# Linear attention and two MLP layers in one kernel: the first layer's groups of three chunks become groups of 2, 4, 4, 4, 4, 4, 2

## What is computed

```python
for t in range(S):
    cur = np.einsum('bhd,bhe->bhde', u[None] * kt, vt)
    y[:, :, t] = np.einsum('bhd,bhde->bhe', rt, state + cur)
    state = w[None, :, :, None] * state + np.einsum('bhd,bhe->bhde', kt, vt)
```

```python
h = np.maximum(np.maximum(x @ w1, x @ w2), x @ w3); x = h @ w_out          # d_ff 768
xn = x / rms * rms_g; out = (silu(xn @ w_gate) * (xn @ w_val)) @ w_out     # d_ff 1536
```

## Time and profile before

| what | us |
|---|---|
| median of three runs | 871.98 (867.09 to 873.14) |
| the profiled execution, its own time | 867.5 |
| its span, first to last instruction | 865.8 |
| granted TensorE clock, mean over the span | 0.996 of 2.4 GHz |

### The profile page before, as it was taken

One profiled execution on the slowest core, in us unless ns is written; L12 is line 12 of the kernel. 1 busy time (PEld: TensorE's weight loads), 2 busy tenths in 40 slices (PEclk: granted clock), 3 DMA queues, 4 the chain that ended last, 5 costly groups with the idle time before them and its releaser, 6 DMA issues.

```text
span 865.8 us, 14428 instructions
## 1 busy us (share of the span) xinstructions
PE 838.9 (97%) x5480; PEld 734.3 (85%) x5480; DVE 361.6 (42%) x665; ACT 314.1 (36%) x684; POOL 148.7 (17%) x148
## 2 busy tenths in 40 slices
PE   3799999999999999999999999999999999999998
PEld 2599999999999999999788888888888888888886
DVE  7675445445535545335333423522433252343221
ACT  3743434243434334343545232332332323233212
POOL 6652321322312321003324000000000000000000
PEclk9899999999999999999999999999999999999999
DMA  6643123113213121032221000000000000000000
GB/s 236 200 162 111 54 68 92 57 59 104 59 53 111 53 79 33 4 96 73 57 71 37 1 37 1 0 37 1 1 22 14 0 0 36 0 0 37 0 1 37
DMA packets 45157, 45.40 MB, mean 52 GB/s; under 512 B 3504, under 2 KB 39728, under 8 KB 45104
## 3 DMA queue, kind: packets, MB, share of 16 engines
q1 hardware_dynamic: 45104, 44.65, 16.4%
HBM read 38.74 MB, written 4.72 MB: 50 GB/s over the span
## 4 chain that ended last, share of the span: by engine, by line
PE 93%; DVE 3%; ACT 1%; issue 1%; DMA 1%; SPq 1%; DVEq 0%; ACTq 0%
PE h_b L442 12%; PE h_b L444 11%; PE h_b L443 11%; PE h2y_b L442 8%; PE h2y_b L444 8%; PE h2y_b L443 8%; PE y_b L444 6%; PE y_b L442 6%; PE y_b L443 6%; PE at_b L403 3%; PE at_b L429 3%; PE at_b L444 3%; PE at_b L442 3%; PE at_b L443 3%; PE at_b L424 1%
## 5 line engine op out<-in xcount | busy, mean ns | idle before, releaser
L442 PE MATMUL h_b<-xh,Wh 128*128 128x384 f32 (+1 forms) x396 | 144.4, 365 | 1.3 <-DVE hB L857 1.3
L444 PE MATMUL h_b<-xh,Wl 128*128 128x384 f32 (+1 forms) x396 | 139.2, 352 | 0.0
L443 PE MATMUL h_b<-xl,Wh 128*128 128x384 f32 (+1 forms) x396 | 139.0, 351 | 0.0
L753 ACT CAST hh<-hB 128x512 fp32r<-128x512 f32 x72 | 44.7, 621 | 163.0 <-DVE hB L1019 160.9
L748 ACT ACTIVATE hA<-h_b 128x512 f32<-128x512 f32 x72 | 43.1, 598 | 125.6 <-PE h_b L444 125.6
L444 PE MATMUL y_b<-hh,Wl 128*128 128x512 f32 (+1 forms) x240 | 88.2, 367 | 0.0
L442 PE MATMUL y_b<-hh,Wh 128*128 128x512 f32 (+1 forms) x240 | 88.1, 367 | 0.0
L443 PE MATMUL y_b<-hl,Wh 128*128 128x512 f32 (+1 forms) x240 | 88.1, 367 | 0.0
L442 PEld LDWEIGHTS h_b<-xh,Wh 128*128 128x128 f32 x396 | 74.7, 189 | 10.4 <-issue 2.8
L1019 DVE TENSOR_TENSOR hB<-h2y_b,hA 128x512 f32<-128x512 f32 x36 | 24.9, 691 | 137.5 <-PE h2y_b L444 137.5
L605 ACT ACTIVATE A<-hA,cur 128x128 f32<-128x128 f32 x192 | 60.6, 390 | 53.5 <-DVE cur L808 36.8
(11 more groups left out here) (151 smaller groups left out, 1553.3 us busy)
## 6 DMA issues: line engine op xcount, KB each, us to landing
kbuf<-in_kT SPq DMA_DIRECT2D x24, 256.0 KB, 3.5
rbuf<-in_rT SPq DMA_DIRECT2D x24, 256.0 KB, 3.5
rnbuf<-in_r SPq DMA_DIRECT2D x24, 192.0 KB, 2.5
knbuf<-in_k SPq DMA_DIRECT2D x24, 192.0 KB, 3.1
vbuf<-in_v SPq DMA_DIRECT2D x24, 192.0 KB, 3.6
x<-in_wA SPq DMA_DIRECT2D x6, 768.0 KB, 6.7
out_t<-xraw SPq DMA_DIRECT2D x5, 768.0 KB, 3.7
wst<-in_gv SPq DMA_DIRECT2D x6, 384.0 KB, 3.2
```

Of the source, the lines that this page charges most:

```text
L442: nc.tensor.matmul(bank[:, 0:n], hi, xhi, start=first, stop=False)
L443: nc.tensor.matmul(bank[:, 0:n], hi, xlo, start=False, stop=False)
L444: return nc.tensor.matmul(bank[:, 0:n], lo, xhi, start=False, stop=last)
L753: nc.scalar.copy(hh[:, f % 2, :], hB[:, f % 2, :]).then_inc(g_hi, 1)
```

## The change

Chunks c and slots q are now counted through the whole run (q = 2c and 2c + 1). Loops of layer 1 are written out.

```diff
-GC = 3
+SIZES = (2, 4, 4, 4, 4, 4, 2)
+NG = len(SIZES)
+STARTS = [sum(SIZES[:g]) for g in range(NG)]
+RING = 3
-SLOTS = (("w1",), ("w1",), ("w1",), ("w1",), ("w1", "out"), ())
+PLACES = {0: (),
+          4: ((0, "w1"), (1, "w1"), (2, "w1"), (3, "w1")),
+          8: ((0, "w1"), (1, "w1"), (1, "w3"), (2, "w3"), (3, "w1"), (3, "w3"), (4, "w1"), (4, "out"))}
+PLACES_0 = ((0, "out"), (1, "w1"), (1, "out"), (2, "w3"), (3, "w1"), (3, "w3"), (4, "w1"), (4, "out"))
+        ident = sb(att, "ident", [P, P])
+        mask = sb(att, "mask", [P, C])
+        p3 = sb(att, "p3", [P, max(SIZES), C])
```

```diff
 SyncE: loads and moves
-            for j in range(GC):
-                load_chunk(0, 0, j)
+            load_chunk(0)
+            load_chunk(1)
             load_wA(0)
             load_wA(1)
-            load_chunk(0, 1, 0)
+            load_chunk(2)
             load_wA(2)
-            move_p3(0, 0)
+            move_p3(sp, 0, HOLES[:3])
+            load_chunk(3)
             load_wA(3)
-            load_chunk(0, 1, 1)
+            load_chunk(4)
             load_wA(4)
             load_wA(5)
 GpSimd: prologue; the low parts of weights go
-            pool.wait_ge(u_loaded, 16)
-            for k in range(Q):
-                prep_r(0, 0, k, first=k < DUOS, following=(0, 1))
-                if k == 0:
-                    wA_low(1)
-                if k == 1:
-                    wA_low(2)
+            prep_r(0)
+            prep_r(1)
+            scale_k(0)
+            prep_r(2)
+            scale_k(1)
+            prep_r(3)
+            pool.wait_ge(u_loaded, 16)
+            current(SIZES[0])
 ScalarE: prologue
+            for q in range(Q0):
+                if q + 2 < Q0:
+                    diagonal(q + 2)
+                take_y(q, FIRST[q % 3])
+                if q == 1:
+                    wA_high(0)
+                if q == Q0 - 2:
+                    move_p3(act, 0, HOLES[3:])
             for c in range(KC):
-                x_high(0, 0, c)
+                x_high(0, c)
+            wA_high(1)
 ScalarE: group and tail
-                    if first and f + 3 < F1:
-                        for third in range(3):
-                            wA_high(f + 3, third)
                     copy_w1(g, f)
+                    if g == 0 and f == 0:
+                        diagonal(Q0)
+                        diagonal(Q0 + 1)
                     slot_work(f, "w1")
                     slot_work(f, "w2")
                     hidden_hi(g, f)
+                    slot_work(f, "w3")
                     slot_work(f, "out")
+                    if g == 0 and f + 2 < F1:
+                        wA_high(f + 2)
+                if f == 4:
+                    normed_high(0, PAR2)
                 for piece in EARLY_SPLITS[f]:
                     split_high(*piece)
-                if f == 4:
-                    normed_high(0, 0)
 VectorE: slot_work and group
+                if q + 1 < NQ:
+                    place_scores(q + 1, at_b)
+                sum_state(q, at_b)
+                if q % 2 == 0 and q // 2 + 1 < NCH:
+                    sum_current(q // 2 + 1)
+                if q + 2 < NQ:
+                    prep(q + 2)
                         if part == "w2":
+                            if g == 0 and f + 1 < F1:
+                                wA_low(f + 1)
                             maximum(g, f, 1)
 VectorE: prologue
             nc.vector.tensor_tensor(pw[:, 7, :], pw[:, 6, :], pw[:, 6, :], ALU.mult)
+            first_current(0)
             then(nc.vector.reciprocal(ipw[:], pw[:, 0:6, :]))
...
+            prep(0)
+            sum_current(0)
             nc.vector.tensor_tensor(PKw, PK[:, :, :].rearrange("p (h m) c -> p h m c", h=2),
...
             dve.wait_ge(consts_ready, 2)
-            prep(0, 0, 0)
-            sum_current(0, 0, 0)
-            prep(0, 0, 1)
-            place_scores(0, 0, 0, FIRST[0], 3)
+            prep(1)
+            first_current(1)
+            place_scores(0, FIRST[0], 3)
+            sum_current(1)
 VectorE: tail, layer 2's first norm
-                if f == 3:
+                if (f, part) == (3, "out"):
                     reciprocal_rms(0)
-                    normalise(0)
-                if f == 4:
-                    normed_low(0, 0)
+                if (f, part) == (4, "out"):
+                    normalise(0)
+                    normed_low(0, PAR2, (0,))
+                if (f, part) == (5, "w2"):
+                    normed_low(0, PAR2, (1, 2))
```

More of the change, by code:

```diff
@@ L652, in group @@
+            def group(g, tail=None):
+                work = slots(g)
+                def slot_work(f, part):
+                    if (f, part) in work:
+                        q = work[f, part]
+                        if q + 2 < NQ:
+                            diagonal(q + 2)
+                        take_y(q, at_b)
                 for f in range(F1):
-                    if f == F1 - 1 and ai is not None:
+                    if f == F1 - 1 and g + 1 < NG:
                         for c in range(KC):
-                            x_high(ai, apar, c)
@@ L886, in wA_low, with group @@
+            def wA_low(f, thirds=(0, 3)):
+                dve.wait_ge(wA_hi, 3 * f + thirds[1])
+                n = W1F // 3
+                cut = slice(f * W1F + n * thirds[0], f * W1F + n * thirds[1])
                 last = nc.vector.tensor_tensor(Wl[:, cut], wraw[:, cut], Wh[:, cut].bitcast(F32), ALU.subtract)
[L887 removed]
+                if thirds[1] == 3:
                     last.then_inc(wA_lo, 1)
[L890 to L893 removed]
+            def group(g, tail=None):
+                work = slots(g)
```

544 lines of the change are left out of this document (244 added, 300 removed).

## The result

In 16 executions of each, on the same chip, the kernel before took 869.91 us (867.09 to 873.14) and the changed one 876.56 us (873.36 to 878.15): a ratio of 1.0078, with a 95% interval from 1.0061 to 1.0094. It is slower by 0.8%, 6.7 us; the forecast was 2.0 above the 871.98 known then. The profiled execution has a span of 875.4 us (before 865.8, forecast 867.8), and a mean granted clock of 0.986. The two profiled executions are not the median ones: the one of before (867.5 us) lies 2.4 us under its median, that of the change (877.18) 0.6 over. So the spans are 9.6 us apart where the medians are 6.7 apart, and what follows accounts for the 9.6.

The account below looks back on a forecast made before the run. TensorE's stream was taken as the bound, busy for 97% of the span. 28.1 + 48.5 + 4 x 63.3 - 1.0 + 56.1 + 35.0 = 419.9 us, layer 2 -0.5, span 867.8, median about 874.0; range 859 to 886.

Parts of the forecast that it names:

- Group sizes: Layer-1 matmuls: 256 columns take 0.120 us each, so all layer-1 products cost 296.7 us, a gain of 2.7 us.
- Rival (b): Layer 1: weight loads set the pace of 256-column matmuls, at 0.173 us each the time is 887 us; chance 0.07.
- Slots and middle groups: Layer 1: two more slots in the groups +3.6 us, joined slots -1.2; a four-chunk group takes 63.3 us without stall.
- rival (e): Middle groups: eight slots don't fit, a miss of 1 us in each of five groups, 879 us; chance 0.10 with (d).
- Prologue: Start of the first group: two chunks instead of three bring the first product to 28.1 us, 9.1 us earlier.
- Rival (d): Start of the first group: the prologue gains nothing beyond 33 us, 879 us; chance 0.10 together with (e).
- First group: First 256-column group: 39.9 us of work plus 8.6 of TensorE waits, 48.5 us in all.
- rival (c): First group: the clock falls in its waits, 19 us more, half absorbed, 884 us; chance 0.05.
- Last group: Last 256-column group: 27.3 us of work plus waits of 1.9, 1.7 and 4.1, sum 35.0 us.
- Layer 2: After layer 1: layer 2 changes by one project, -0.5 us.
- The sum: Whole kernel: layer 1 ends at 419.9 us, where 417.42 was; span 867.8 us, median about 874.0.
- (a): First and last groups: waits stay at lower bounds, -6.2 and -4.4 us, 863.4 us; chance 0.28.

Follow-up runs that it names:

- all3: Changed kernel with eight groups of three chunks, its other edits kept and loads and slot places fitted: 872.74 us, ratio 1.0047.
- cur_pool: Changed kernel with first_current undone, GpSimd again making the products of chunks 0 and 1 in the prologue: 877.67 us, ratio 1.0111, four executions.
- fill_first: Changed kernel with idle 256-column matmuls in three TensorE waits: behind the prologue and ahead of two first-group slots: 872.91 us, ratio 1.0038.
- norm_early: Changed kernel with layer 2's first norm begun one group earlier: 865.71 us, ratio 0.9973.
- fill_end: Changed kernel with 20 idle 512-column matmuls ahead of TensorE's wait for the last maximum before layer 2: 873.57 us, ratio 1.0035.
- last3: Changed kernel with group sizes (2, 4, 4, 4, 4, 3, 3), so three chunks in the last group: 867.78 us, ratio 0.9993.
- gate_split: Changed kernel with TensorE's wait ahead of layer 2 divided, only the value products waiting for the last maximum: 873.7 us, ratio 1.0033.
- y_first: Changed kernel with ScalarE's take_y put ahead of the diagonals in the groups' slot work: 872.17 us, ratio 1.0044.
- first6: Changed kernel with sizes (2, 3, 4, 4, 4, 4, 3), so six slots in the first group: 867.63 us, ratio 0.9983.
- early_y_first6: Changed kernel with the edits of norm_early and y_first and the sizes of first6: 860.26 us, ratio 0.9905.

## Why the prediction was right, and where it wasn't

The time fell into the forecast's case (874.0 forecast, 876.56 measured, own range 866 to 880), within 1% of before and on its slow side. That closeness is partly luck. The 874.0 stood on a median of three, 871.98, which is 869.91 in 16 executions; the change itself was forecast at +2.0 us and measured at +6.7, and the span's sum missed 7.6 us. The range was wide enough for that. What failed is one mechanism, the clock behind TensorE's waits, which the sum put at nothing. By the steps of the prediction:

- **Group sizes: held.** 256 columns take 0.120 us, as assumed. Rival (b), loads that set the pace, is out. The five middle groups take 308.2 us, forecast 308.3.
- **Slots and middle groups: held.** There is no wait in 308 us, so rival (e), slots that don't fit, is out. Joining the rows of slots seems worth 0.4 us per group in all3, which has the other edits too, against the 0.2 assumed.
- **Prologue: held.** First product at 27.76, forecast 28.1. The copies were issued until 25.8 on ScalarE and 26.1 on SP, and the casts follow:

```profile
23.95 1.88 ACTq L241 DMA_DIRECT2D xraw<-p  x3
23.95 2.15 SPq L241 DMA_DIRECT2D xraw<-p  x3
...
27.44 0.71 ACT L621 CAST xh<-xraw 128x256 fp32r<-128x256 f32 x2 [0.29 <-DMA xraw<-p]
```

  What cur_pool adds: without first_current it would be 30.2. Rival (d) is out.
- **First group: two errors that half cancel.** The forecast was 39.9 of work and 8.6 of waits, 48.5; it was 51.0, inside the 45 to 52 that the prediction allowed. The waits are 4.7. At full clock they would be more, up to 6.6 by fill_first (its fillers and idle time together): the low clock stretches the parts between slots, and the chain behind a slot gains time by that. The step that failed is in rival (c), "against: the longest wait I find there is 3 us". A wait of 2.15 us was followed by 6.3 us at the lower level, and the prologue's pause, which I knew to end in a slow product, by 3.5 us of it, which the sum did not hold at all. 46.15 us busy at 0.87 are 40.1 at full clock, the forecast's 39.9: the work was sized right, and 6.0 us of clock were left out. fill_first shows the cause: with the clock kept up the group takes 3.6 us less. Rival (c) thus happened in part; its price of 19 us, half absorbed, was for a clock that stays down, and it came back each time. The rows of before held the term already: the 2.4 us that the prediction took from the first group of before as waits are 0.44 us of idle time (49.22 less 48.78) and 48.78 x 0.04 = 2.0 us of clock.
- **Last group: mis-sized by 2.9.** 35.0 forecast, 37.9 measured. Waits 2.07, 1.62 and 4.67 (forecast 1.9, 1.7, 4.1), so 0.7 of it; the rest is mostly the 1.8 us of clock behind the wait of 2.07. The mechanism, copy_w1(5) behind a cast and two normed_low ahead of the second maximum, is the one forecast. What the forecast did not see is that the norm need not wait for this group: norm_early took 7.5 us out of it.
- **Layer 2: wrong sign.** -0.5 forecast, +2.1 measured. The pause of 4.67 us in front of it was forecast within 0.6, yet its consequence for the clock was not drawn, although show a slow product behind a pause of this size. fill_end takes exactly this out: 447.9.
- **The sum.** 867.8 forecast, 875.4 measured: -0.3 at the start, +2.5 in the first group, -0.1 in the middle, +2.9 in the last group, +2.6 in layer 2. The spread of the change's executions fits the clock as its cause, though no run isolates it: the fastest two, 873.36 and 873.83 us, ran at 0.994 and 0.996, the slowest two at 0.986 and 0.988. In the kernel before the recorded clock does not order them: at 1.00 there are executions of 867.6 us and of 871.7.
- **The chances.** "Half of (a) and its better end, 0.27" doesn't come out: (a) has 0.28 in all and its time, 863.4, lies at the 1% line, so half of it is 0.14.
- **The other parts.** That only one group is short of cover is shown by last3 and norm_early: either alone brings the change to the time of before or just below. all3 shows that the other edits are not free with groups of three chunks: 3.9 us by span, from the first group and the start of layer 2.

Still open: which pause is followed by a fall. The one of 2.06 us in the last group was followed by one in two of six profiled executions (after, fill_first; not in fill_end, gate_split, cur_pool, y_first), the one of 3.1 us in first6 and all3 and not in last3, though TensorE had been busy without a pause since 400 us in first6 and last3 alike. No run isolates it.

## What to carry to other kernels

Price a wait on TensorE twice: its own length, and the work behind it at half speed; here a wait of about 2 us cost from nothing to 3 us more behind it, and one of 4.7 us 2.6 more. When a group becomes shorter, count what it covered, and begin that work one group earlier before making the group longer. In a queue in order, put the instruction that another engine waits for ahead of those that nobody needs yet: swapping two calls brought the ratio from 1.0078 to 1.0044.

## What the hardware showed that I had not expected

- The clock can fall behind a wait of 2 us. The largest pauses without slow products behind them were 1.88 us (y_first), 2.06 us (four executions), 2.25 us (early_y_first6) and 3.10 us (last3); with slow products behind them were 1.83, 2.07 and 2.15 us (after), 2.46 us (norm_early), 3.11 us (first6, all3), and those of 4.67 in all four profiles that have one. The Trainium skill, TensorE: Matmul & The Clock Gate, section Why this matters for your kernels, warns of idle gaps between bursts, but only of longer ones than the waits inside the first group; by that these would have been harmless, and the runs decide against it.
- A low stretch lasted 3.5 us at the first group's start, 6.3 us behind its wait and 5.7 us at the start of layer 2, with TensorE busy all the time. In early_y_first6 the first three products behind the prologue's pause are fast, and those from 28.5 to 35.1 us slow, so that the best version still loses some 3 us there (an estimate: half of the stretch, as each product takes twice its time).
- The recorded clock can be wrong: it is 1.00 in the prologue of y_first, whose products take 0.63 us where they take 0.39 at full clock.
- Matmuls whose results nobody uses keep the clock up: no slow products through the first group of fill_first, nor at the start of layer 2 of fill_end.
- 256 columns of float32r with a weight load each take 0.120 us, though the rows of the loads show 0.188 us or more each: in the rows successive loads overlap.
- VectorE's cast of 0.50 us took 1.90 beside GpSimd's products in cur_pool, as the k product did before; by cur_pool, a product moved from GpSimd to VectorE can cost less than it takes.
